# Issuing the first stage's weight loads from the scalar engine's queue instead of the sync engine's

## The reference

```python
# attention, per token t (state starts at 0)
cur = einsum('bhd,bhe->bhde', u[None] * kt, vt)
y[:, :, t] = einsum('bhd,bhde->bhe', rt, state + cur)
state = w[None, :, :, None] * state + einsum('bhd,bhe->bhde', kt, vt)
# first block: w_in is 384 x 2048, w_out is 2048 x 384
h = x @ w_in
g = where(h >= 1, h, where(h <= -1, 0, (h + 1) ** 2 / 4))
x = g @ w_out
# second block: 8 experts, each 384 x 1024 x 384, gate from a softmax over normalised logits
```

## Time and profile before

| | |
|---|---|
| median of 3 runs | 820.4 us |
| profiled execution, its own time | 818.09 us |
| its span | 816.3 us |
| PE busy | 755.1 us (92%) |
| DVE busy | 426.5 us (52%) |
| ACT busy | 299.8 us (37%) |
| POOL busy | 149.2 us (18%) |
| mean granted TensorE clock | 0.974 of full speed |

### The profile page before, as it was taken

How to read it: one execution, slowest core, us unless ns; L and a number is a source line. 1 busy time by engine, 2 the same in 40 slices (tenths; PEclk the granted TensorE clock), 3 DMA queues, 4 the chain that set the end, 5 groups by cost and what they waited for, 6 DMA issues and landing times. The chain is left out here.

```text
span 816.3 us, 12482 instructions
## 1 busy us (share of the span) xinstructions
PE 755.1 (92%) x4840; PEld 617.5 (76%) x4841; DVE 426.5 (52%) x676; ACT 299.8 (37%) x489; POOL 149.2 (18%) x166
## 2 busy tenths in 40 slices
PE   4778999999999999999999999999549999999995
PEld 3656887778878687778878688868239998998985
DVE  5779864664656464664656464644254323223232
ACT  2355443533454343533454343634233112121120
POOL 6534732121222222121222200000070000000000
PEclk9799999999999999999999999999859999999998
DMA  9981112111111112110100000000170202202021
GB/s 153 256 163 31 30 30 52 45 21 21 30 59 30 30 30 58 41 23 17 31 40 1 0 2 40 1 0 1 62 249 1 79 1 78 68 11 77 0 77 39
DMA packets 87931, 40.34 MB, mean 49 GB/s; under 512 B 76728, under 2 KB 84544, under 8 KB 87872
## 3 DMA queue, kind: packets, MB, share of 16 engines
q1 hardware_dynamic: 86560, 34.81, 17.7%
q10 hardware_dynamic: 1312, 4.73, 1.5%
HBM read 30.10 MB, written 9.44 MB: 48 GB/s over the span
## 5 line engine op out<-in xcount | busy, mean ns | idle before, releaser
L792 PE MATMUL x_ps<-g_p,wout_hi 128*128 128x512 f32 x576 | 184.7, 402 | 3.5 <-DVE g_p L621 3.2
L806 PE MATMUL h_ps<-x0T,win_hi 128*128 128x512 f32 x576 | 180.3, 394 | 1.2 <-DVE x0T L548 1.2
L432 ACT ACTIVATE above<-h_ps,minus_one 128x512 f32<-128x512 f32 x96 | 66.1, 688 | 210.0 <-DVE mid L630 209.5
L630 DVE TENSOR_SCALAR mid<-h_ps 128x512 f32<-128x512 f32 x96 | 66.2, 689 | 131.7 <-PE h_ps L806 131.5
L792 PEld LDWEIGHTS x_ps<-g_p,wout_hi 128*128 128x128 f32 x576 | 103.4, 188 | 35.3 <-issue 8.1
L806 PEld LDWEIGHTS h_ps<-x0T,win_hi 128*128 128x128 f32 x576 | 107.5, 189 | 24.0 <-DVE x0T L548 1.5
L1337 PE MATMUL ch_ps<-x_p,w_p 128*128 128x512 f32 x432 | 109.3, 401 | 11.8 <-DVE w_p L1403 11.8
L806 PE MATMUL h_ps<-x0T,win_lo 128*128 128x512 f32 x288 | 113.0, 392 | 0.0
L792 PE MATMUL x_ps<-g_p,wout_lo 128*128 128x512 f32 x288 | 112.6, 391 | 0.0
L634 DVE TENSOR_TENSOR mid<-mid,above 128x512 f32<-128x512 f32 x96 | 77.2, 804 | 67.5 <-ACT mid L433 67.5
L1326 PE MATMUL cy_ps<-w_p,h_p 128*128 128x384 f32 x576 | 107.8, 336 | 0.0
(11 more groups left out here) (186 smaller groups left out, 656.1 us busy)
## 6 DMA issues: line engine op xcount, KB each, us to landing
xr<-xT_scratch SPq DMA_DIRECT2D x8, 768.0 KB, 4.9
rkv<-in_r SPq DMA_DIRECT2D x24, 192.0 KB, 3.1
rkv<-in_k SPq DMA_DIRECT2D x24, 192.0 KB, 3.8
rkv<-in_v SPq DMA_DIRECT2D x24, 192.0 KB, 2.8
xT_scratch<-xbuf ACTq DMA_DIRECT2D x6, 768.0 KB, 3.3
out<-acc SPq DMA_DIRECT2D x12, 384.0 KB, 2.5
wout_raw<-in_moe_w_out SPq DMA_DIRECT2D x4, 768.0 KB, 13.3
raw<-in_moe_w SPq DMA_DIRECT2D x8, 384.0 KB, 6.8
```

What stands on the lines that cost most here:

```text
L432: raises(act.activation(above[:, f % 2], h_ps[f % 2][:, :], ACT.Relu, bias=minus_one[:, :]), "over")
L630: raises(dve.tensor_scalar(mid[:, f % NM], h_ps[f % 2][:, :], -1.0, 1.0, ALU.max, ALU.min), "clamped")
L792: last = pe.matmul(x_ps[kk][:, :], (wout_hi, wout_lo)[a][:, f, cols], g_p[:, f % NG, b], start=(f == 0 and n == 0), stop=(f == NF1 - 1 and ...
L806: last = pe.matmul(h_ps[f % 2][:, :], (win_hi, win_lo)[a][:, f // QF, kk, cols], x0T[:, c % 2, b, kk], start=(kk == 0 and n == 0), stop=(k ...
```

## The change

`load_win` and `load_wout` move from SP's instruction list into ACT's, with their bodies unchanged. ACT issues `load_win(0)` and `load_wout(0)` after its small loads and ahead of the copy to `tab_r`, and the rest after that copy and ahead of the first `turned_rk`. SP goes from `load_v(3)` straight to tile 4.

```diff
@@ block.sync
                 load_rk(3)
                 load_v(3)
-                load_win(0)
-                load_wout(0)
-                load_win(1)
-                for i in range(1, NQ):
-                    load_wout(i)
                 for it in range(B, NTILE):
                     load_rk(it)
                     load_v(it)
@@ block.scalar
+                def load_win(i):
+
+                    some = slice(0, 1) if i == 0 else slice(1, NQ)
+                    for kk in range(KD):
+                        for s in range(4):
+                            pr, strip = (2 * kk + s // 2, s % 2 * 2) if kk < 2 else (s, 1)
+                            act.dma_start(win_raw[s * HALF:(s + 1) * HALF, some, kk, :],
+                                         w_strips[pr, strip][:, some, :]).then_inc(win_loaded[i], 16)
+
+                def load_wout(i):
+                    rows = slice(i * QF, (i + 1) * QF)
+                    act.dma_start(wout_raw[:, rows, :], wout_v[:, rows, :]).then_inc(wout_loaded[i], 16)
...
                 act.dma_start(tau_e[:, :], tau.rearrange("(a o) -> a o", a=1).broadcast_to([E, 1])).then_inc(emb_loaded, 16)
+                load_win(0)
+                load_wout(0)
                 act.wait_ge(powers_turned, 1)
                 act.activation(flat(tab_r[:, :, :]), x_ps[0][:, 0:HD], ACT.Copy).then_inc(tab_r_done, 1)
+                load_win(1)
+                for i in range(1, NQ):
+                    load_wout(i)
                 turned_rk(0, set_a, first_turn[0], 2)
```

More of the change, by code:

```diff
@@ L270, in load_v @@
                     sp.dma_start(rkv[:, b, 2], v_v[b, n]).then_inc(v_loaded[b], 16)
[L272 to L283, removed]
                 load_rk(0)
```

## The result

The changed kernel takes 831.15 us, the median of four runs (827.42 to 832.26), against 820.45 us for the kernel before (819.95 to 820.97). By the medians it is 10.7 us slower; the ratio of the means is 1.0122 with a 95% interval of 1.0089 to 1.0155, which is 7.3 to 12.7 us. The profiled execution took 830.61 us, with a span of 828.8 us.

What follows compares the result with a forecast made beforehand. The opening's chain over four tiles was taken to set the main loop's start, with PE bound afterwards. 16.2 - 2.1 = +14.1 us on 818.09 us gave 832.2 us, plus 2.3 us to the median 834.5 us; range 821.5 to 838.5 us.

Steps and rivals of the forecast that it cites:

- the case that was held likeliest: Opening: DMA engines alternate packets between the two queues, slowing token loads; 833.0 to 836.0 us, chance 0.45.
- Step 1: Opening, ACT's list: thirteen issues ahead of the table load make tab_r start at 11.74 us, 2.95 us late.
- Step 2: Opening, ACT's list: fifteen more issues put the first rT at 21.98 us instead of 13.55 us.
- Step 3: Opening: token loads share DMA engines with weights; k of tile 2 lands at 33.1 to 36.1 us, 16.2 us taken.
- Step 4: Tile 4's turn: its loads no longer wait behind the weights, so PE waits less; 2.1 us come back.
- The second item: Behind tile 4's stall: a shorter stall may avoid the lowered clock; up to 1.7 us, counted as 0.
- equal time: Opening: both queues get half the engines' time, weights drain slower and hold ACT, rT about 29 us; 828.9 us, chance 0.23.
- The tokens keep their pace: Opening: token loads are not slowed, only ACT's issue time counts; +1.4 us, 821.8 us, chance 0.19.
- The faster rival: Tile 4 early and clock kept give 3.8 us back, start moves under 2.2 us; 818.6 us, chance 0.05.
- The fourth rival: Opening: weights hold ACT longer than SP, besides late tokens, making ACT last again; beyond 838 us, chance 0.08.

Runs made afterwards that it cites:

- a4: Changed kernel with 192 KB `w_in` strips and `w_out` quarters each cut within the runs into two transfers, packets half as long: 829.88 us, ratio 1.0122.
- d1: Changed kernel with 24 instead of 12 transfers for the rest of `w_in`, two per `w_out` quarter, cut between full-length runs: 829.00 us, ratio 1.0104.
- second profile: Kernel before and changed kernel each run once more, unedited, for another profile: 819.26 us and 831.19 us.
- a1: Kernel before with r and k of tile 4 issued by SP ahead of the weights, v behind them: 817.01 us against 819.91 us, ratio 0.9963.
- a2: Kernel before, weights still on SP, plus 28 small transfers issued by ACT in the changed kernel's places: 820.58 us against 819.91 us, ratio 1.0006.
- b1: Kernel before with only the 13 weight issues ahead of tab_r moved to ACT: 819.22 us against 819.61 us, ratio 0.9994.
- a3: Changed kernel with all ACT-issued weights moved behind the first four copies (rT, kT, rT_b, kT_b): 822.80 us against 819.91 us, ratio 1.0029.

## Why the prediction was right

It was right in its direction and its main mechanism; 834.5 us was forecast, 831.15 us measured, inside the range and 3.35 us off. In the terms of the sum, +14.1 us was forecast and +10.7 us measured by the medians. The time of 831.15 us is below the 833.0 to 836.0 us of the case that was held likeliest, and at the low end of the 831 to 837 us given for that case with the clock's return.

- **Step 1** (tab_r at 11.74 us): measured 11.74 us. The experiment with small issues has it at 11.69 us with next to no traffic, so this step is the issue time alone.
- **Step 2** (rT at 21.98 us): measured 24.31 us. The hold of the last three issues was 7.55 instead of 4.05 us; that the weights drain more slowly beside the tokens fits this, but no run tests it alone. Against that, three of the twelve strips were issued beside the table load, and the nine behind tab_r took 4.52 instead of 5.70 us. It lay off the path, as step 3 said. a4 shows where it comes onto it: with rT at 33.8 us.
- **Step 3** (k of tile 2 at 33.1 to 36.1 us, merge 14.7 to 17.7 us late, 16.2 us taken): measured 33.9 us and 15.6 us. The pair a4 and d1 shows that the tokens' pace follows the length of the weights' runs and not the number of transfers, as turns by packets have it; until then that was only an argument. The turns are not strictly one for one: in 7.8 us with 231 GB/s some 49 long packets per engine passed beside 64 short ones, and in a4 in 4.8 us some 53 of half the length (estimates from the bytes moved). The rule of the Trainium skill in "DMA: Bandwidth & Descriptors", section "Queues, rings and completion order", agrees with these runs in kind. What the same page of the Trainium skill says in its section "Issuing engines are not separate DMA queues", that transfers of all issuers interleave on the same 16 engines, agrees too: the token loads on SP's queue slowed down beside ACT's. The prediction drew from these sections that nothing is won in bandwidth; the page of the changed kernel has 187 instead of 153 GB/s in the first slice, which fits the long packets in it; the loads that the start waited for had nothing of it.
- **The merge and the start**: step 3 took the start to be as late as the merge. It was 14.6 us late instead of 15.6 us, since the stretch from the merge to the start took 18.6 instead of 19.5 us. Here too the clock is in it: the granted clock of the kernel before was 0.74 and 0.61 in this stretch, and in its second profile, with 0.50 between 30 and 36 us, the stretch took 20.5 us. The prediction took the stretch as fixed. Its end in the kernel before:

```profile
38.63 1.08 PE L725 MATMUL a_ps<-sc_m,vz 128*32 128x128 f32 x16
39.65 1.35 PE L692 MATMUL h_ps<-rkv,ks_b 128*128 128x96 f32 x8
```

  and in the changed kernel, with the window around it:

```profile
54.48 1.10 PE L692 MATMUL h_ps<-rkv,ks_b 128*128 128x96 f32 x8 [1.39 <-DVE sc_m_b L527]
...
54.00:58.00 4.00, 2.32 (x41) 1.98 (x42) 2.55 (x7) 1.34 (x2) 0.29 (x2) 1.00 0.85 159
```

  Before, PE was still at tile 2's products when the merge of tile 3 ended at 38.5 us, and began tile 3's state update 1.1 us later; in the changed kernel it stood waiting and began 0.15 us after the merge.
- **Step 4** (2.1 us back): measured 2.2 us, and a1 gives them without the change. The second item, up to 1.7 us of clock, was counted at 0. The drop behind tile 4's stall is gone in the changed kernel, in a1, a2, a3, a4, b1 and d1, but in the changed kernel that was worth 0.6 us, because PE then waited for ACT's copy.
- **The sum**: against the first profile of before, 14.6 - 2.2 - 0.6 = 11.8 us at tile 5's turn; with the clock that this profile kept behind tile 5 it is 13.3 us at tile 6's turn, and 12.5 us at the end. The second profiles give 13.8 - 2.1 - 0.6 = 11.1 us at both turns, and 11.9 us at the end. What shifts the rest by 0.8 us either way behind tile 6 was not followed. The 3.35 us by which the forecast was high add up as follows. It was high by 1.6 us in the delay of the start (0.6 us in the merge, 1.0 us in the stretch behind it), by 0.1 us in the wait and by 0.6 us in the clock, 2.3 us up to tile 5's turn. Behind it the profiled pair fell apart by another 0.8 us (1.6 us of clock, less the 0.8 us), which takes the excess to 1.6 us. The other 1.8 us come from the last step: the forecast added the whole distance of 2.3 us between the profile of before and the median, while the changed kernel's profile lay only 0.5 us below its own median. The mechanism was right, and its sizes erred mostly to one side; the range, 17 us wide, was what took it in. That the other runs of the kernel before have both drops is inferred from their median and the second profile; they have no trace.

The rival "equal time" expected POOL to wait little and rT near 29 us: both absent. "The tokens keep their pace" is what a2 and a3 made of it, at 820.6 and 822.8 us. The faster rival needed a start less than 2.2 us late; even with only small issues (a2) it was 3.9 us late. The fourth rival, a deeper hold of ACT, came half true: the hold was deeper (7.55 instead of 4.05 us), but ACT was not last, and in a4, where it was, the time was 829.88 us and not beyond 838 us.

## What to carry to other kernels

A second queue is not a second road: before moving long-packet transfers to another engine, look at which short-packet loads are on the way at that time, and who waits for the last of them. Prefer to reorder within one queue: here two small loads ahead of the bulk were worth 2.9 us, while the bulk on its own queue cost 10.7 us. Read the granted clock behind every stall that an edit removes or adds, but don't book it in full: look at what the engine would wait for at the full clock. Take a second profile if the first lies off the median.

## What the runs showed of the hardware

- A load of 1024 packets of 192 bytes went from 0.99 us to 6.8 and 7.8 us beside 2 KB packets of the other queue, and to 4.2 and 4.8 us beside 1 KB packets.
- A full queue holds the engine that issues: three `wout` issues took 7.55 us in the changed kernel and six took 10.08 us in a4, in which ACT did nothing else.
- A delay of the start of 3.7 to 3.9 us (b1, a2) cost between -0.4 and +0.7 us in all, because a stall of 3.0 us behind it shrank (to 0.8 us in b1, to 1.7 us in a2), and with the stall the drop of the clock went.
- A lowered clock costs what PE's work was the limit for: 0.79 over 8 us cost about 0.6 us behind tile 4's turn, where PE at the full clock waits 1.33 us for ACT, and 1.6 us behind tile 5's, where PE is busy throughout.
